# RWKV attention with two MLP blocks on one core: the bonus term of y moves from TensorE transposes to the diagonal of the masked scores on VectorE, for tiles 6 to 11

## The reference

```python
def _attn_ref(r, k, v, w, u):
    for t in range(S):
        cur = np.einsum('bhd,bhe->bhde', u[None] * kt, vt)
        y[:, :, t] = np.einsum('bhd,bhde->bhe', rt, state + cur)
        state = wt[:, :, :, None] * state + np.einsum('bhd,bhe->bhde', kt, vt)

def _moe_ref(x, w_in, conv_w, w_out):          # 384 -> 1024 -> 384
    h = np.maximum(x @ w_in, 0.0)
    ...                                        # conv_out: 3 taps over the steps of h
    gate = 1.0 / (1.0 + np.exp(-conv_out))
    return h * gate @ w_out

def _moe2_ref(x, g_ln, w_ch1, w_ch2):          # 384 -> 1536 -> 384
    xn = (x - mu) / np.sqrt(var + 1e-06) * g_ln
    return x + np.maximum(xn @ w_ch1, 0.0) @ w_ch2
```

## Time and profile before

| | before |
|---|---|
| median of 3 runs | 345.92 us (345.42 to 348.71) |
| the profiled execution | 345.48 us |
| its span | 343.7 us |
| TensorE busy | 331.6 us, 96% |
| VectorE busy | 245.3 us, 71% |
| ScalarE busy | 138.7 us |
| GpSimd busy | 69.6 us |
| granted clock of TensorE | full in all 40 slices |
| mean DMA share | highest in the first 10 slices, under a half in most later ones |

### The profile page before, as it was taken

The page is one execution under the profiler, slowest core; times in us unless marked ns, Lnnn a source line. Parts: engine busy times, 40 slices in busy tenths (PEclk is TensorE's granted clock), DMA queues, the critical chain, the costliest instruction groups (busy, mean ns, idle before and its releaser), DMA issues.

```text
span 343.7 us, 8530 instructions
## 1 busy us (share of the span) xinstructions
PE 331.6 (96%) x3184; PEld 310.8 (90%) x3184; DVE 245.3 (71%) x525; ACT 138.7 (40%) x333; POOL 69.6 (20%) x160
## 2 busy tenths in 40 slices
PE   7987999999999999999999999999999999999996
PEld 6866768999998899999899999899999999998996
DVE  4997789899897777597867598787785612766222
ACT  2225864635474222374212275312374322753110
POOL 5654001242402032000322110332130100100100
PEclk9999999999999999999999999999999999999999
DMA  9968625913144320344521353140000100000101
GB/s 154 221 127 257 212 72 170 256 30 55 18 76 70 50 69 5 42 49 65 116 51 19 44 88 48 51 82 2 2 3 1 47 0 2 0 2 1 49 0 46
DMA packets 89251, 22.79 MB, mean 66 GB/s; under 512 B 83423, under 2 KB 87674, under 8 KB 89210
## 3 DMA queue, kind: packets, MB, share of 16 engines
q1 hardware_dynamic: 87984, 21.84, 31.7%
q10 hardware_dynamic: 1226, 0.41, 0.7%
HBM read 19.87 MB, written 2.36 MB: 65 GB/s over the span
## 4 chain that ended last, share of the span: by engine, by line
PE 77%; DVE 4%; issue 1%; ACT 0%; DVEq 0%; ACTq 0%
PE hid L618 12%; PE hid L619 11%; PE hid L622 11%; PE acc L630 7%; PE acc L631 7%; PE acc L638 3%; PE acc L637 3%; PE pair_a L1377 2%; PE pair_a L630 2%; PE pair_a L631 2%; PE y_ps L1414 2%; PE pair_a L637 2%; PE pair_b L631 2%; PE pair_b L638 2%; PE pair_b L630 2%; DVE stats L1264 1%
## 5 line engine op out<-in xcount | busy, mean ns | idle before, releaser
L1055 ACT ACTIVATE g_hi<-hid 128x256 fp32r<-128x256 f32 x58 | 22.2, 384 | 93.9 <-PE acc L638 80.8
L618 PE MATMUL hid<-xc_hi,w_hi 128*128 128x256 f32 x216 | 54.9, 286 | 1.1 <-DVE xc_lo L1276 0.6
L1296 DVE SCALAR_TENSOR_TENSOR g_lo<-hid,g_hi 128x256 fp32r<-128x256 f32 x58 | 24.4, 420 | 43.0 <-ACT g_hi L1055 42.9
L1076 DVE SCALAR_TENSOR_TENSOR cg<-h_all,cols,cg 128x256 f32<-128x256 f32 x96 | 46.1, 481 | 9.8 <-ACT cg L1021 8.9
L619 PE MATMUL hid<-xc_hi,w_lo 128*128 128x256 f32 x216 | 53.0, 277 | 0.0
L618 PEld LDWEIGHTS hid<-xc_hi,w_hi 128*128 128x128 f32 x216 | 40.6, 188 | 3.7 <-issue 1.4
L619 PEld LDWEIGHTS hid<-xc_hi,w_lo 128*128 128x128 f32 x216 | 40.6, 188 | 0.0
L630 PE MATMUL acc<-w_hi,g_hi 128*128 128x384 f32 x116 | 40.1, 345 | 0.0
L618 PE MATMUL hid<-x_hi,win_hi 128*128 128x258 f32 (+1 forms) x144 | 38.4, 296 | 1.2 <-POOL x_hi L886 1.2
L631 PE MATMUL acc<-w_lo,g_hi 128*128 128x384 f32 x116 | 39.1, 337 | 0.0
L619 PE MATMUL hid<-x_hi,win_lo 128*128 128x258 f32 (+1 forms) x144 | 36.7, 283 | 0.0
(11 more groups left out here) (195 smaller groups left out, 759.8 us busy)
## 6 DMA issues: line engine op xcount, KB each, us to landing
v_in<-in_v SPq DMA_DIRECT2D x12, 192.0 KB, 3.1
lent<-in_moe_w_ch SPq DMA_DIRECT2D x6, 384.0 KB, 5.1
lent<-in_moe_w_in SPq DMA_DIRECT2D x6, 256.0 KB, 4.5
lent<-in_moe_w_out SPq DMA_DIRECT2D x4, 384.0 KB, 7.3
w_two<-in_w SPq DMA_DIRECT2D x6, 192.0 KB, 6.2
k_two<-in_k SPq DMA_DIRECT2D x6, 192.0 KB, 4.6
bv<-in_k SPq DMA_DIRECT2D x6, 192.0 KB, 3.1
ruk<-in_r SPq DMA_DIRECT2D x6, 192.0 KB, 3.0
```

Source lines behind the costliest of these rows:

```text
L618: pe.matmul(out_ps, wh, xh, start=i == 0, stop=False)
L1055: act.activation(relu_parts(n, j)[0], hid[j % 2][:, 0:GP], ACT.Relu)\
L1076: dve.scalar_tensor_tensor(out=cv, in0=h[:, t:t + GP], scalar=cols[:, t * JF + j:t * JF + j + 1], in1=cv, op0=ALU.mult, op1=ALU.add).then_ ...
L1296: dve.scalar_tensor_tensor(out=low, in0=hid[j % 2][:, 0:GP], scalar=0.0, in1=high.bitcast(F32), op0=ALU.max, op1=ALU.subtract).then_inc(s_ ...
```

## The change

For tiles n >= `DIAGONAL_FROM` = 6:

- `bv` is no longer GpSimd's. VectorE does it: eight instructions, one for each head, each of which reads the 128 x 128 identity, a column of `bonus` as a scalar for each partition, and the 128 x 128 block of `scores`, and writes the block back with the bonus added on its diagonal. It waits for `bonus` and for the masked scores.
- `y` has no transposes. The first matmuls into each region of `y_ps` open it with `start`: those of the state, or in tile 6 those of the scores. The wait for `bv` comes behind the state's matmuls, ahead of the scores'.
- `bonus` has two buffers; `sums` waits one tile less. Tiles 0 to 5 stay as they were, but for that.
- Items of `AFTER` stand elsewhere. Because VectorE now does `bv` behind `mask`, it is moved to a place behind `mask` in each tile. Other items are moved too: `kv` of tile 7 from behind `turn` of group 2 to behind the first `hidden2` of it; `sc` of tile 9 ahead of a `project2`; `y` and `x` of tile 9 one `project` later, with `x` behind `scan1` of tile 10; `ke` of tile 10 behind two more `project2`; `kv` and `state` of tile 10 into group 4's first block.

```diff
-        bonus = sb("bonus", [P, H])
+        bonus = [sb("bonus0", [P, H])]
...
-            ("project2", 1, 2): [("ru", 7), ("bv", 6)],
+            ("project2", 1, 2): [("ru", 7)],
             ("hidden2", 1, 5): [("mask", 6)],
-            ("project2", 1, 3): [("w", 7), ("ruk", 7), ("middle", 7), ("sc", 6)],
+            ("project2", 1, 3): [("w", 7), ("ruk", 7), ("bv", 6), ("middle", 7), ("sc", 6)],
...
-                elif kind == "bv":
+                elif kind == "bv" and n < DIAGONAL_FROM:
                     bonus_values(n)
...
                 elif kind == "sums":
                     dve.wait_ge(s_ruk, n + 1)
-                    if n:
-                        dve.wait_ge(s_bv, n)
-                    dve.reduce_sum(bonus[:, :], by_head(ruk), AX.X).then_inc(s_bonus, 1)
+                    if n >= 2:
+                        dve.wait_ge(s_bv, n - 1)
+                    dve.reduce_sum(bonus[n % 2][:, :], by_head(ruk), AX.X).then_inc(s_bonus, 1)
+                elif kind == "bv" and n >= DIAGONAL_FROM:
+                    dve.wait_ge(s_bonus, n + 1)
+                    dve.wait_ge(s_sc, 2 * (n + 1))
+                    for a in range(PAIRS):
+                        for e in range(2):
+                            on = scores_of(n)[:, a, e, :]
+                            last = dve.scalar_tensor_tensor(out=on, in0=ident[:, :],
+                                                            scalar=bonus[n % 2][:, 2 * a + e:2 * a + e + 1],
+                                                            in1=on, op0=ALU.mult, op1=ALU.add)
+                    last.then_inc(s_bv, 1)
...
-                    pe.wait_ge(s_bv, n + 1)
-                    for a in range(KD):
-                        pe.matmul(y_ps[:, a * P:(a + 1) * P], bv[n % 2][:, a * P:(a + 1) * P], ident[:, :],
-                                  start=a == 0, stop=False, is_transpose=True, skip_group_check=True)
+                    on_diagonal = n >= DIAGONAL_FROM
+                    if not on_diagonal:
+                        pe.wait_ge(s_bv, n + 1)
+                        for a in range(KD):
+                            pe.matmul(y_ps[:, a * P:(a + 1) * P], bv[n % 2][:, a * P:(a + 1) * P], ident[:, :],
+                                      start=a == 0, stop=False, is_transpose=True, skip_group_check=True)
+
+                    opening = set()
+                    if on_diagonal:
+                        opening = set(range(4)) if n % SEQ else {0, 2, 3, 5}
...
                     pe.wait_ge(s_sc, 2 * (n + 1))
+                    if on_diagonal:
+                        pe.wait_ge(s_bv, n + 1)
```

More of the change, by code:

```diff
@@ L411, in rwkv_mlp_kernel @@
             ("turn", 1): [("late", 0, 11), ("scan1", 6)],
+            ("hidden2", 1, 2): [("sums", 6)],
             ("project2", 1, 0): [("scan2", 6)],
-            ("hidden2", 1, 3): [("sums", 6), ("r", 6), ("x", 5)],
+            ("hidden2", 1, 3): [("r", 6), ("x", 5)],
             ("project2", 1, 1): [("row_k", 7), ("mid", 6)],
             ("hidden2", 1, 4): [("row_r", 7)],
-            ("project2", 1, 2): [("ru", 7), ("bv", 6)],
+            ("project2", 1, 2): [("ru", 7)],
             ("hidden2", 1, 5): [("mask", 6)],
-            ("project2", 1, 3): [("w", 7), ("ruk", 7), ("middle", 7), ("sc", 6)],
+            ("project2", 1, 3): [("w", 7), ("ruk", 7), ("bv", 6), ("middle", 7), ("sc", 6)],
             ("hidden2", 1, 6): [("r", 7)],
@@ L422, in rwkv_mlp_kernel @@
             ("project2", 1, 6): [("x", 6), ("load_k", 8), ("k", 7), ("mid", 7)],
-            ("hidden2", 1, 9): [("bv", 7)],
             ("hidden2", 1, 10): [("sums", 7), ("state", 6), ("mask", 7)],
             ("project2", 1, 8): [("kv", 6), ("sc", 7)],
+            ("hidden", 2, 0): [("bv", 7)],
             ("conv", 2, 0): [("load_w", 8), ("ke", 7)],
@@ L435, in rwkv_mlp_kernel @@
             ("norm", 2): [("scan1", 8)],
-            ("turn", 2): [("kv", 7)],
-            ("result", 1): [("ru", 9)],
+            ("result", 1): [("ru", 9), ("kv", 7)],
             ("hidden2", 2, 1): [("scan2", 8)],
-            ("project2", 2, 0): [("r", 8), ("state", 7)],
+            ("project2", 2, 0): [("r", 8)],
             ("hidden2", 2, 3): [("mid", 8)],
-            ("project2", 2, 1): [("sums", 8)],
+            ("project2", 2, 1): [("state", 7), ("sums", 8)],
             ("hidden2", 2, 4): [("load_v", 8)],
-            ("project2", 2, 2): [("mask", 8), ("middle", 8)],
+            ("project2", 2, 2): [("mask", 8), ("bv", 8), ("middle", 8)],
             ("add", 1, 0): [("ruk", 9), ("row_k", 9)],
@@ L446, in rwkv_mlp_kernel @@
             ("project2", 2, 4): [("r", 9), ("ke", 8)],
[1 row of a table removed]
+            ("hidden2", 2, 7): [("sums", 9)],
             ("project2", 2, 5): [("k", 9), ("w", 9)],
             ("hidden2", 2, 8): [("scan1", 9), ("scan2", 9), ("row_r", 9)],
[2 rows of a table removed]
+            ("project2", 2, 7): [("mid", 9)],
+            ("hidden2", 2, 10): [("load_v", 9), ("y", 8), ("x", 8)],
+            ("hidden2", 2, 11): [("sc", 9), ("mask", 9), ("bv", 9)],
             ("conv", 3, 0): [("state", 8), ("load_w", 10)],
@@ L457, in rwkv_mlp_kernel @@
             ("project", 3, 2): [("ru", 10)],
-            ("conv", 3, 7): [("row_r", 10), ("r", 10), ("y", 9)],
-            ("project", 3, 4): [("x", 9), ("load_k", 10)],
-            ("gate", 3, 7): [("scan1", 10)],
+            ("conv", 3, 7): [("row_r", 10), ("r", 10)],
+            ("project", 3, 4): [("load_k", 10)],
+            ("gate", 3, 7): [("y", 9), ("scan1", 10), ("x", 9)],
             ("project", 3, 7): [("ke", 9), ("ruk", 10)],
@@ L468, in rwkv_mlp_kernel @@
             ("project2", 3, 3): [("w", 11), ("r", 11), ("scan1", 11)],
[1 row of a table removed]
+            ("hidden2", 3, 6): [("row_k", 11), ("mask", 10), ("bv", 10), ("sums", 11)],
             ("hidden2", 3, 7): [("sc", 10), ("scan2", 11), ("k", 11)],
             ("project2", 3, 5): [("x", 10)],
[1 row of a table removed]
+            ("project2", 3, 6): [("mid", 11), ("ke", 10), ("y", 10), ("load_v", 11)],
             ("hidden2", 3, 9): [("row_r", 11)],
[2 rows of a table removed]
+            ("hidden2", 3, 10): [("mask", 11), ("sc", 11)],
+            ("hidden", 4, 0): [("bv", 11)],
             ("hidden", 4, 1): [("late", 3, 8)],
-            ("gate", 4, 0): [("bv", 11)],
+            ("hidden", 4, 3): [("kv", 10)],
+            ("gate", 4, 2): [("state", 10)],
             ("project", 4, 4): [("y", 11)],
@@ L1414, in _ @@
                             pe.matmul(rows_32(i), state[n % 2][0:ROW1, i // 3, 32 * (i % 3):32 * (i % 3) + 32],
-                                      r_mid[n % 2][0:ROW1, i // 3, :], start=False, stop=False,
+                                      r_mid[n % 2][0:ROW1, i // 3, :], start=i in opening, stop=False,
                                       skip_group_check=True)
+                        opening = set()
                     pe.wait_ge(s_sc, 2 * (n + 1))
+                    if on_diagonal:
+                        pe.wait_ge(s_bv, n + 1)
                     for i in range(HD // 32):
@@ L1420, in _ @@
                             pe.matmul(rows_32(i), v_in[b][:, 32 * i:32 * i + 32],
-                                      scores_of(n)[:, i // 3, i % 3 // 2, :], start=False, stop=False,
+                                      scores_of(n)[:, i // 3, i % 3 // 2, :], start=i in opening, stop=False,
                                       skip_group_check=True)
```

4 lines of the change are left out of this document (3 added, 1 removed), and 7 rows, old and new, of the table AFTER.

## The result

| | before | after |
|---|---|---|
| median | 345.83 us (345.41 to 348.71, 11 runs) | 348.87 us (346.89 to 351.91, 11 runs) |
| ratio after : before, 95% | | 1.0072 (1.0049 to 1.0095) |
| profiled execution, its span | 345.48, 343.7 us | 348.73, 347.0 us |

The account below looks back on a forecast made before the run. It took TensorE's own work and waits as the bound. Its terms, -2.0 + 0.5 + 0.5 + 0.2 + 0.7 + 0.2, gave +0.1 us, thus 345.8 us, with a range of 344.0 to 348.5.

Parts of the forecast that it names:

- transposes, for each y: TensorE loses three transposes in each of six tiles: 0.42 us less 0.09 for the switch, -2.0 us in all.
- the eight: VectorE's eight diagonal instructions: 0.27 us from start to start, 0.35 for the last, 2.2 us a tile, 13 in all.
- tile 6: TensorE, without transposes, reaches L1420 early and waits for the eight until 129.87: +0.5 us.
- tile 7: The eight fit into VectorE's 2.26 us wait ahead of group 2's first taps: 0.
- tile 8: The eight, from 178.23 to 180.45, delay a low part that TensorE's hidden2 (2, 7) needs: +0.5 us.
- tile 9: Mask and eight end at 196.77, so the taps start at 196.69 instead of 196.49: +0.2 us.
- tile 10: The low part slips 2.2 us, but hidden2 (3, 9) starts later because y stands before it: 0.
- tile 11: Group 4's first taps move about 0.4 us; kv of tile 10 ahead of project (4, 0) gives 0.7 us: 0.
- kv 7: kv of tile 7 leaves a hole at turn 2 for a place where TensorE is full: +0.7 us.
- turn 3: At norm 3 the statistics start about when they did, so part of tile 9's gain is taken back: +0.2 us.
- the clock: TensorE's granted clock: the prediction's sum had no term for a fall of it.
- rival 3: The eight run at half rate, a block of 3.3 us: about +6 us, 352 us; chance 6%.

Follow-up runs that it names:

- e2: The changed kernel with DIAGONAL_FROM = 12: new order and two bonus buffers kept, transposes and GpSimd's bonus values in all tiles; 346.91 us, ratio 1.0035.
- e6: e1 with kv of tile 7 put back behind turn 2; 345.23 us, ratio 0.9988 against the kernel before.
- e1: The changed kernel plus one wait holding GpSimd's products of tile 9 until VectorE's eight of tile 8 are done; 345.92 us, ratio 1.0004.
- e5: A small separate kernel: VectorE's eight alone 2.19 us, beside three GpSimd products 4.49, beside products with the identity in PSUM 2.16.
- e7: The kernel before's order with bv moved behind mask, the diagonal from tile 6, and GpSimd held as in e1; 348.81 us, ratio 1.0067.

## Why the prediction was wrong, and where it was right

| step | forecast, us | in the traces |
|---|---|---|
| transposes, for each y | -0.33 | -0.33 (7), -0.34 (8), -0.37 (10), -0.33 (11) |
| the eight | 0.35 each, 2.2 a tile | 0.347, 2.15 to 2.19 in five tiles |
| tile 6 | +0.5 | a wait of 0.47; with the transposes +0.2 |
| tile 7 | 0 | 0; 0.16 us left ahead of the taps |
| tile 8 | +0.5 | **+2.1** |
| tile 9 | +0.2 | +0.24 |
| tile 10 | 0 | 0 |
| tile 11 | 0 | +0.3, of which 0.2 are in e2 too |
| kv 7 | +0.7 | +0.67, and 0.6 to 0.8 back in e6 |
| turn 3 | +0.2 | -0.1 |
| sum behind 26 us | +0.1 | +1.6 |
| the clock | no term | **+1.5** in the profiled run, early |

- **The term that failed is tile 8.** "the eight run from 178.23 to 180.45" had the right start and waits, but the 0.27 us an instruction came from places where GpSimd is quiet. I bounded the instruction by its own overlap (0.20 to 0.35) and not by its neighbour: two of the eight took 1.10 and 1.08 us, and the group 3.72 instead of 2.2. The 0.5 was right for the kernel without the encounter: in e1 it is 0.55, and e1's 345.85 at full clock is +0.15 against before, where my sum says +0.1.
- **The clock was put at nothing**, by "I keep the clock of the trace before". That trace was one without a fall. The changed kernel fell in 20 of 23 runs, 1.5 us for each fall, and that is the other half of the 3 us: its median is 348.87, its three runs at full clock have 347.28, 1.6 above before.
- **The half rate** of rival 3 didn't come: 0.347 us each, alone as in the kernel. What really spoke against the change were the two engines meeting, 2.30 us more for three products in e5, and the prediction has no term for that.
- **Turn 3 and tile 11** were off by 0.3 each and cancel. I had judged both by single distances, as the prediction's last sentence warned. e7 shows how near the edge they stand: there slips of the same kind cost 1.3 us at tile 9 and 1.1 at group 4.
- **The range** was made of costs at full clock. The three runs shown, 345.42 to 348.71, already held a spread of 3.3 us for one kernel, and I took only "what the spread of runs takes" off the chance. Even with tile 8 as it is, the changed kernel takes 347.28 us at full clock, inside the range; the falls, in 20 of 23 runs, put the median above it.
- The size of the loss, 0.7%, is within 1%, as 91% of the chance had it. But it came by two causes of which the prediction names neither.

## What to carry to other kernels

Before work moves to VectorE with two sources in SBUF, lay GpSimd's rows of the same stretch beside it: each GpSimd instruction that meets it can hold up one of VectorE's (here 0.77 us for a product of 1.0 us, 0.26 for a copy), and the trace shows the price wherever two such already meet. A single wait on the engine that isn't in a hurry (GpSimd) removed it. A new stall of TensorE as long as these (1.6 and 1.8 us) is to be priced twice, once as itself and once for the clock that may fall behind it; the ones of 1.2 to 1.4 us brought no fall in any trace here. And a forecast for a median needs the share of falling runs, before and after, not only the costs at full clock. And items in the order that look like mere shuffling can be what makes the main edit free, so undo them one at a time.

## What was not expected of the hardware

- VectorE and GpSimd alternate one for one: 0.34 us became 1.07 beside a product of 1.0 us, and nothing was lost with one source in PSUM (2.16 us for eight). GpSimd's single-source copy holds VectorE up as well (3.50 for 2.19). A pair takes less than its two lengths: 1.4 us for 0.69 and 1.0.
- The same hole of 1.6 us is followed by 1.2 GHz for 3.4 us in some executions (1.5 us lost) and by 2.4 GHz in others. One microsecond of dummy matmuls 4 us ahead of the hole stopped that in 24 runs of 24, without filling it.
